# A second PSUM bank for the attention's output in the first half of a kernel

## The chip, the cores and the metric

The kernel runs on one core of a Trainium2 chip. The metric is the time on the device of one execution, in microseconds. In this text PE is TensorE (matmuls), DVE is VectorE, ACT is ScalarE, POOL is GpSimd and SP is the engine that issues the loads and stores.

## What is computed

Three layers follow one another. The first is a decayed linear attention over 4 batches, 8 heads, 768 positions and a head size of 64; the second and third are feed-forward layers over the 3072 tokens that come out of it.

```python
# attention, per batch and head
state = gamma * state + outer(k[t], v[t])
y[t] = q[t] @ state / sqrt(D)
# second layer, x is (3072, 512)
h = x @ w_in                                 # (3072, 1024)
e = exp(h - max(h)); solu = h * e / sum(e)
ln = (solu - mean(solu)) / sqrt(var(solu) + 1e-6) * g_ln
x2 = ln @ w_out                              # (3072, 512)
# third layer
h2 = x2 @ w2_in                              # (3072, 2048)
out = (h2 * cos(h2)) @ w2_out
```

## The kernel before

**Two halves.** The first half computes the attention and the second layer, the second half computes the third layer. The change touches the first half alone. It works on tiles of 128 tokens, six to a batch (TILES), 24 in all, and each tile has all eight heads as four pairs.

**Two parts for each number.** Each operand is split in a high part and a low rest, both of the type that PE multiplies fast. `products` issues three matmuls for each product: high by high, high by low and low by high. Names ending in _h are written by ACT as a copy, names ending in _l by DVE or POOL as the whole less the high part. In the rows L321, L323 and L324 are those three matmuls, whatever the product is, so that the names of the operands tell which product it is.

**The attention of a tile.** SC multiplies queries and keys (operands q and k, 12 matmuls). DVE masks the result into p_m (L1116), ACT copies it to p_h (L786) and DVE subtracts to get p_l (L1123), each for two groups g of two head pairs. DL makes the state's products in `ps_d`. ST (DVE) updates the state s, SH and SL split it. O0 and O1 multiply p by v and, for all but the first tile of a batch, q by the state: that is the output of group 0 and of group 1, 12 matmuls each, 6 for the first tile of a batch. ACT copies each group out of PSUM to x_h (L795) and DVE subtracts from PSUM to get x_l (L1149).

**The second layer of a tile.** L1a and L1b (12 matmuls each, operands w1i and x) make h in two banks. L1a waits for x_l of the tile, and for the step U of the tile before, since the bank of h is read there. DVE takes the maximum (nmax, L1169), ACT the exponential (L813), U on DVE multiplies (L1175). CEN subtracts the mean, T0 and T1 transpose on PE (L627), L2a and L2b (18 and 6 matmuls, operands w1o and z) multiply by w_out, YT transposes the result (L662).

**The order.** Every engine walks the same list of steps, STEP, written out by hand, in which each step has a number of tiles by which it lags. For a middle turn of the loop PE's share of it is SC, T0, L1b, DL, T1, O0, L2a, O1, YT, L2b, after the turn's own L1a. The first turns have lists of their own (`head`), and steps whose tile doesn't exist yet are left out: L2a lags by three turns, so in the turns of tiles 0 and 1 nothing of PE stands between O0 and O1. In these turns ACT and DVE also split the weights of the second layer (step W1: ACT L802 and L808, DVE L1158 and L1163), and DVE does the subtractions that POOL does later (by_dve, q_l at L1107 among them). Each engine takes its instructions strictly in the order of the list, and waits on semaphores.

**The eight banks of PSUM in the first half.** `ps_p` and, in the same two banks, `ps_d`: 0 and 1. `ps_o`: 2. Bank 3: nothing. `ps_h`: 4 and 5. `ps_t`: 6. `ps_y`: 7. In the second half `ps_out` is banks 2 to 7.

**The wait in question.** O0 and O1 write the same bank, so each waits until the x_l of the group before it has been read. The third argument of `wait` from the end is how many counts a tile has, the last the index in the tile; a value that is not positive makes no wait.

```python
g = int(name == "O1")
wait(pe, pl_done, b, t, 2, g)
wait(pe, xl_done, b, t, 2, g - 1)
```

Of the kernel before, what the change touches and what calls it, by code (L numbers as in the profile page):

```python
# [94 lines left out]
def build(nc, qT, kT, kn, vn, consts, w1_in, w1_out, g_ln, w2_in, w2_out, y_scratch, w2_split,  # L95
          w2o_split, out):
    ctx = ExitStack()
    with ctx:
# [2 lines left out]

        bank = ctx.enter_context(nc.psum_tensor("bank", [128, 8, 512], F32))
        ps_p = bank[:, 0:2, :]
        ps_o = bank[:, 2, :]

        ps_d = bank[:, 0:2, :].rearrange("p g (j a n) -> p (g j) a n", j=2, a=2)
        ps_h = bank[:, 4:6, :]
# [103 lines left out]
        xh_done, xl_done = sem("xh_done"), sem("xl_done")  # L211
# [76 lines left out]
        def wait(eng, s, batch, tile, per=1, i=0, per_batch=TILES):  # L288


            value = batch * (per_batch * per) + (tile * per + i + 1)
            if not isinstance(value, int):
                assert value.min_val >= 1
                eng.wait_ge(s, value)
            elif value > 0:
                eng.wait_ge(s, value)
# [20 lines left out]
        def products(eng, dst, terms, first, last_one, read_between=False):  # L317

            n = len(terms)
            for i, (ah, al, bh, bl) in enumerate(terms):  # L320
                eng.matmul(dst, ah, bh, start=first and i == 0, stop=False,  # L321
                           skip_group_check=read_between)
                eng.matmul(dst, ah, bl, start=False, stop=False, skip_group_check=read_between)  # L323
                m = eng.matmul(dst, al, bh, start=False, stop=last_one and i == n - 1,  # L324
                               skip_group_check=read_between)
            return m

        def two_pairs(x):

            return x.rearrange("p (j a t) -> p j a t", j=2, a=2)  # L330
# [216 lines left out]
        def _(pe):  # L547
            def step(name, t, b):
                par = t % 2
                if name == "SC":  # L550
# [6 lines left out]
                    for g in range(2):  # L557
                        wait(pe, pm_done, b, t - 1, 2, g)
                        for j in range(2):
                            p = 2 * g + j  # L560
                            cols = slice(p * C, (p + 1) * C)
                            m = products(pe, ps_p[:, g, j * 256:(j + 1) * 256], [
                                (k_h[:, par, cols], k_l[:, par, cols], q_of(q_h, par, p),
                                 q_of(q_l, par, p))], True, True)
                        m.then_inc(qk_done, 1)
                elif name == "DL" and t % TILES < TILES - 1:
# [3 lines left out]
                    for p in range(PAIRS):  # L570
                        if p % 2 == 0:
# [4 lines left out]
                        m = pe.matmul(ps_d[:, p, 0, :], n_l[:, par, cols], v_h[:, par, cols],  # L576
                                      start=False, stop=True)
                    m.then_inc(d_done, 1)
                elif name in ("O0", "O1"):

                    g = int(name == "O1")
                    wait(pe, pl_done, b, t, 2, g)
                    wait(pe, xl_done, b, t, 2, g - 1)
                    if g == 0:
                        wait(pe, v_lo, b, t)
                        if t % TILES > 0:
# [1 line left out]
                    for j in range(2):  # L588
                        p = 2 * g + j
                        cols = slice(p * 128, (p + 1) * 128)  # L590
                        o = slice(j * 256, (j + 1) * 256)
                        terms = [(v_h[:, par, cols], v_l[:, par, cols],
                                  p_h[:, g, o], p_l[:, g, o])]
                        if t % TILES > 0:
                            n = (t % TILES - 1) % 2
                            terms.append((s_h[:, n, cols], s_l[:, n, cols],
                                          q_of(q_h, par, p), q_of(q_l, par, p)))
                        m = products(pe, ps_o[:, o], terms, True, True)
                    m.then_inc(o_done, 1)
                elif name in ("L1a", "L1b"):  # L600
                    half = int(name == "L1b")
# [3 lines left out]
                    for k in range(KD):  # L605
                        if isinstance(b, int) and t == 0:
                            pe.wait_ge(w1_lo, k + 1)
                        if half == 0 and k % 2 == 0:
                            wait(pe, xl_done, b, t, 2, k // 2)
                        m = products(pe, ps_h[:, half, :], [  # L610
                            (x_h[:, par, k, :], x_l[:, par, k, :],
                             w1i_h[:, k, cols], w1i_l[:, k, cols])], k == 0, k == KD - 1)
# [147 lines left out]
        def _(act):  # L760
# [3 lines left out]
            def step(name, t, b):  # L764
# [8 lines left out]
                elif name == "PQ":  # L773
                    wait(act, q_sc, b, t)
                    for a in range(2):
                        r = slice(64 * a, 64 * a + 64)
                        m = act.copy(q_h[r, par, :, a, :], raw[r, par, 0, :].rearrange(  # L777
                            "p (c t) -> p c t", c=PAIRS))
                    m.then_inc(q_hi, 1)
                elif name == "PN":  # L780
                    wait(act, n_sc, b, t)
                    act.copy(n_h[:, par, :], raw[:, par, 2, :]).then_inc(n_hi, 1)
                elif name == "SC":
                    for g in range(2):
                        wait(act, pm_done, b, t, 2, g)
                        act.copy(p_h[:, g, :], p_m[:, g, :]).then_inc(ph_done, 1)  # L786
                elif name == "SH" and t % TILES < TILES - 1:
                    wait_state(act, st_done, b, t)
                    act.copy(s_h[:, t % TILES % 2, :], s_32[:, :]).then_inc(sh_done, 1)
                elif name in ("O0", "O1"):  # L790
                    g = int(name == "O1")
                    wait(act, o_done, b, t, 2, g)
                    for a in range(2):
                        r = slice(64 * a, 64 * a + 64)
                        m = act.copy(x_h[r, par, 2 * g:2 * g + 2, :],  # L795
                                     two_pairs(ps_o[r, :])[:, :, a, :])
                    m.then_inc(xh_done, 1)
                elif name == "W1":
                    act.wait_ge(ld_w1[t], 16)
                    w = w1_raw[:, t % W1_SLOTS, :]  # L800
                    if t < KD:
                        act.copy(w1i_h[:, t, :], w).then_inc(w1_hi, 1)  # L802
                    else:

                        act.wait_ge(ld_mask, 32)
                        for n in range(2):
                            k = 2 * (t - KD) + n
                            m = act.activation(w1o_h[:, k, :], w[:, n * 512:(n + 1) * 512],  # L808
                                               ACT.Copy, scale=g_col[:, k:k + 1])
                        m.then_inc(w1_hi, 1)  # L810
                elif name == "EX":
                    wait(act, nm_done, b, t)
                    act.activation(e_b, ps_h[:, :, :].rearrange("p a n -> p (a n)"), ACT.Exp,  # L813
                                   bias=nmax[:, par:par + 1],
                                   accum_out=esum[:, par:par + 1]).then_inc(e_done, 1)
                elif name in ("T0", "T1"):
                    g = int(name == "T1")
                    wait(act, t_done, b, t, 2, g)
                    act.copy(z_h[:, 4 * g:4 * g + 4, :].rearrange("p k t -> p (k t)"), ps_t[:, :])\
                        .then_inc(zh_done, 1)  # L820
                elif name in ("L2b", "LD"):
                    wait(act, l2_done, b, t)
                    wait(act, scl_done, b, t, 2, 1)
                    act.activation(y32, ps_y[:, :], ACT.Copy, scale=scl[:, par, 3:4])\
                        .then_inc(y_done, 1)
                elif name == "SQ":
                    wait(act, nmu_done, b, t)
                    act.activation(e_b, u_b, ACT.Square, bias=nmu[:, par:par + 1],
                                   accum_out=ssq[:, par:par + 1]).then_inc(sq1_done, 1)
                elif name == "WH" and unit(b, t) is not None:  # L830
                    u = unit(b, t)
                    unit_wait(act, s4_done, b, u)
                    unit_wait(act, wi_stored, b, u - 1, 16)
                    act.copy(w_out[:, :, 0, :], w_raw[:, A11:, :]).then_inc(wi_hi, 1)
                    unit_wait(act, ld_wo, b, u, 16)
                    unit_wait(act, wo_stored, b, u - 1, 16)
                    act.copy(wo_out[:, 0, :], wo_raw[:, :]).then_inc(wo_hi, 1)
                elif name == "TBL":
                    act.activation(warm[:, :], mhalf[:, :], ACT.Sin)
                elif name == "YH":  # L840
                    y_hi(0, t)
                elif name == "P":
                    slot(0, 0, t, True)
                elif name == "Q":
                    slot(0, 1, t, True)
# [229 lines left out]
        def _(dve):  # L1075
# [9 lines left out]
            def step(name, t, b):  # L1085
# [58 lines left out]
                elif name in ("O0", "O1"):  # L1144
                    g = int(name == "O1")
                    wait(dve, xh_done, b, t, 2, g)
                    for a in range(2):
                        r = slice(64 * a, 64 * a + 64)
                        m = dve.tensor_tensor(x_l[r, par, 2 * g:2 * g + 2, :],  # L1149
                                              two_pairs(ps_o[r, :])[:, :, a, :],  # L1150
                                              x_h[r, par, 2 * g:2 * g + 2, :].bitcast(F32),
                                              ALU.subtract)
                    m.then_inc(xl_done, 1)
# [261 lines left out]
```

## Time and profile before

| what | value |
|---|---|
| time, median of 3 runs | 953.51 us (953.22 to 953.98) |
| the profiled execution's own time | 953.76 us |
| its span in the profile | 952.0 us |
| PE busy | 924.0 us, 97% |
| DVE busy | 714.0 us, 75% |
| ACT busy | 563.1 us, 59% |
| POOL busy | 294.5 us, 31% |
| mean granted clock of PE | 0.991 |

The span runs from the first to the last instruction that the profile records; 1.76 us of the execution's own time lie around it. An engine's idle time matters only where the chain of work that ends last passes through it. The granted clock is given as a share of 2.4 GHz: 1.00 is the upper of its two levels, 0.50 is the lower, 1.2 GHz. The end of a matmul in the profile is modelled, and one may start before the record of the one ahead has ended: the distance between two starts tells the pace.

### The profile page before, as it was taken

The page shows a single profiled execution, that of the slowest core. Times are in us where ns is not written, and L with a number is a line of the kernel's source. Part 1 is how long each engine was busy: PE and PEld are TensorE (multiplying, and loading weights), DVE is VectorE, ACT ScalarE, POOL GpSimd, SP SyncE. Part 2 cuts the span into 40 slices and gives each one's busy share as a digit, 9 for nine tenths or more (in the row PEclk, how much of TensorE's full clock was granted, in tenths as well). Part 3 has the DMA queues.
Part 4 walks back from the last instruction along what each step waited for, and adds up shares of the span by engine and source line. Part 5 has one row for each costly group of instructions (what it writes and reads, how often), then busy time and mean ns, then how long its engine had stood idle before and what let it go on. Part 6 is the DMA issues. An engine that isn't in the chain of part 4 may idle for free.

```text
span 952.0 us, 14590 instructions
## 1 busy us (share of the span) xinstructions
PE 924.0 (97%) x4912; PEld 819.3 (86%) x4912; DVE 714.0 (75%) x1052; ACT 563.1 (59%) x923; POOL 294.5 (31%) x282
## 2 busy tenths in 40 slices
PE   3799999999999999999999999999999999999998
PEld 3588888888888888888989999999999999999997
DVE  8989799988998798977656586566766566766564
ACT  5656656657657567546645475555665455656453
POOL 2475777777776767751000000000000000000000
PEclk8799999999999999999999999999999999999999
DMA  7423364453463453528796444734446444454301
GB/s 279 156 67 117 101 228 164 159 174 138 183 228 118 162 191 138 202 85 267 250 314 215 115 123 125 241 111 124 114 127 218 148 118 122 113 184 121 110 12 66
DMA packets 106520, 148.18 MB, mean 156 GB/s; under 512 B 7408, under 2 KB 77040, under 8 KB 106480
## 3 DMA queue, kind: packets, MB, share of 16 engines
q1 hardware_dynamic: 106480, 147.69, 47.7%
q8 instruction: 20, 0.33, 0.1%
q14 instruction: 20, 0.16, 0.1%
HBM read 112.01 MB, written 35.65 MB: 155 GB/s over the span
## 4 chain that ended last, share of the span: by engine, by line
PE 88%; DVE 8%; ACT 2%; issue 1%; DMA 1%; POOL 0%; SPq 0%; DVEq 0%; ACTq 0%; POOLq 0%
PE bank L321 28%; PE bank L324 28%; PE bank L323 28%; PE bank L627 2%; DVE p_l L1123 1%; PE bank L662 1%; DVE p_m L1116 1%; PE bank L574 1%; DVE wo_out L1223 1%; DVE s_l L1142 1%; DVE z_l L1203 1%; ACT q_h L777 1%; DVE nmax L1169 1%; DVE w1i_l L1158 0%; DVE x_l L1149 0%
## 5 line engine op out<-in xcount | busy, mean ns | idle before, releaser
L321 PE MATMUL bank<-yc_h,ring 128*128 128x384 f32 x448 | 151.5, 338 | 0.0
L323 PE MATMUL bank<-yc_l,ring 128*128 128x384 f32 x448 | 151.3, 338 | 0.0
L324 PE MATMUL bank<-yc_h,ring 128*128 128x384 f32 x448 | 150.9, 337 | 0.0
L1049 POOL TENSOR_TENSOR y_raw<-y_raw,t 128x768 f32<-128x768 f32 x4 | 7.4, 1854 | 361.2 <-DVE yc_l L1234 361.2
L1252 DVE SCALAR_TENSOR_TENSOR gg<-turns,c 128x768 f32<-128x768 int32 x64 | 61.0, 953 | 63.8 <-ACT turns L866 63.8
L872 ACT ACTIVATE gg<-gg 128x768 f32<-128x768 f32 x64 | 54.2, 846 | 80.2 <-DVE gg L1259 80.1
L866 ACT ACTIVATE turns<-c 128x768 int32<-128x768 f32 x64 | 54.2, 847 | 79.1 <-DVE c L1322 76.6
L321 PEld LDWEIGHTS bank<-yc_h,ring 128*128 128x128 f32 x448 | 84.2, 188 | 7.9 <-issue 0.5
L323 PEld LDWEIGHTS bank<-yc_l,ring 128*128 128x128 f32 x448 | 84.2, 188 | 7.2
L324 PEld LDWEIGHTS bank<-yc_h,ring 128*128 128x128 f32 x448 | 84.1, 188 | 0.0
L321 PE MATMUL bank<-w1i_h,x_h 128*128 128x512 f32 x192 | 78.5, 409 | 4.3 <-DVE x_l L1149 1.8
L982 POOL TENSOR_TENSOR q_l<-raw,q_h 64x512 fp32r<-64x512 f32 x44 | 56.7, 1289 | 65.9 <-ACT q_h L777 62.2
L321 PE MATMUL bank<-w1o_h,z_h 128*128 128x512 f32 x192 | 76.8, 400 | 0.0
L324 PE MATMUL bank<-w1i_h,x_l 128*128 128x512 f32 x192 | 76.0, 396 | 0.0
L323 PE MATMUL bank<-w1i_l,x_h 128*128 128x512 f32 x192 | 75.6, 394 | 0.0
L324 PE MATMUL bank<-w1o_h,z_l 128*128 128x512 f32 x192 | 75.4, 393 | 0.0
L323 PE MATMUL bank<-w1o_l,z_h 128*128 128x512 f32 x192 | 75.1, 391 | 0.0
L324 PE MATMUL bank<-w2o,glo_l 128*128 128x512 f32 x192 | 75.0, 391 | 0.0
L323 PE MATMUL bank<-w2o,glo_h 128*128 128x512 f32 x192 | 75.0, 391 | 0.0
L323 PE MATMUL bank<-w2o,ghi_h 128*128 128x512 f32 x192 | 74.9, 390 | 0.0
L324 PE MATMUL bank<-w2o,ghi_l 128*128 128x512 f32 x192 | 74.8, 390 | 0.0
L321 PE MATMUL bank<-w2o,glo_h 128*128 128x512 f32 x192 | 74.6, 389 | 0.0
(129 smaller groups left out, 2471.9 us busy)
## 6 DMA issues: line engine op xcount, KB each, us to landing
ring<-w_split SPq DMA_DIRECT2D x224, 256.0 KB, 2.8
w_split<-w_out SPq DMA_DIRECT2D x16, 896.0 KB, 6.4
w2o_split<-wo_out SPq DMA_DIRECT2D x16, 512.0 KB, 5.5
w2o<-w2o_split SPq DMA_DIRECT2D x8, 1024.0 KB, 7.7
raw<-kT SPq DMA_DIRECT2D x24, 256.0 KB, 2.6
raw<-qT SPq DMA_DIRECT2D x24, 256.0 KB, 2.9
raw<-kn SPq DMA_DIRECT2D x24, 256.0 KB, 3.9
raw<-vn SPq DMA_DIRECT2D x24, 256.0 KB, 4.8
```

The lines of the kernel that those rows point to most:

```text
L321: eng.matmul(dst, ah, bh, start=first and i == 0, stop=False, skip_group_check=read_between)
L323: eng.matmul(dst, ah, bl, start=False, stop=False, skip_group_check=read_between)
L324: m = eng.matmul(dst, al, bh, start=False, stop=last_one and i == n - 1, skip_group_check=read_between)
L574: pe.matmul(ps_d[:, p, :, :], n_h[:, par, cols], v_hl[:, :, par, cols], start=True, stop=False)
L627: m = pe.transpose(ps_t[:, k * 128:(k + 1) * 128], c_b[:, (4 * g + k) * 128:(4 * g + k + 1) * 128], ident[:, :])
L662: m = pe.transpose(ps_t[:, k * 128:(k + 1) * 128], y32[:, k * 128:(k + 1) * 128], ident[:, :])
L777: m = act.copy(q_h[r, par, :, a, :], raw[r, par, 0, :].rearrange("p (c t) -> p c t", c=PAIRS))
L866: act.activation(turns[:, r, :], flat(c_32[:, r, :, :]), ACT.Copy, scale=INV_2PI)\
L872: act.activation(gg[:, r, :], gg[:, r, :], ACT.Sin, scale=0.5)\
L982: return pool.tensor_tensor(dst, whole, part.bitcast(F32), ALU.subtract)
L1116: dve.tensor_tensor(two_pairs(p_m[:, g, :]), two_pairs(ps_p[:, g, :]), mask[:, 4 * g:4 * g + 4, :].rearrange("p (j a) t -> p j a t", j=2), ...
L1252: dve.scalar_tensor_tensor(gg[:, r, :], turns[:, r, :], -TWO_PI_HI, flat(c_32[:, r, :, :]), ALU.mult, ALU.add)\
```

## The change

`ps_o` becomes two banks, 2 and 3. Group 0 (O0) stays in bank 2 and group 1 (O1) goes to bank 3. PE's wait now asks for the read of the same group of the tile before, where it asked for the group before. Counted from the start of the run, O of group g of tile t waited for 2t + g reads and waits for 2t + g - 1. ACT and DVE read the bank of their group. Nothing is moved, no instruction is added that does work, no transfer changes.

```diff
-        ps_o = bank[:, 2, :]
+        ps_o = bank[:, 2:4, :]
...
                     wait(pe, pl_done, b, t, 2, g)
-                    wait(pe, xl_done, b, t, 2, g - 1)
+                    wait(pe, xl_done, b, t - 1, 2, g)
...
-                        m = products(pe, ps_o[:, o], terms, True, True)
+                        m = products(pe, ps_o[:, g, o], terms, True, True)
...
-                                     two_pairs(ps_o[r, :])[:, :, a, :])
+                                     two_pairs(ps_o[r, g, :])[:, :, a, :])
...
-                                              two_pairs(ps_o[r, :])[:, :, a, :],
+                                              two_pairs(ps_o[r, g, :])[:, :, a, :],
```

## Rows read from the trace of the kernel before

**Rows 1.** The page, busy time, share of the span and instructions of each engine.
```profile
...
PE 924.0 (97%) x4912; PEld 819.3 (86%) x4912; DVE 714.0 (75%) x1052; ACT 563.1 (59%) x923; POOL 294.5 (31%) x282
...
```

**Rows 2.** The waits of PE: waited for, us in total, times, longest.
```profile
...
PE bank L321 <- DVE x_l L1149: 8.0, 6, 2.9
PE bank L321 <- DVE p_l L1123: 3.8, 5, 1.9
...
```

**Rows 3.** The timeline of PE, 14 to 49 us: start, us, instruction, [idle before <- releaser].
```profile
...
17.05 0.28 PE L324 MATMUL bank<-p_h,v_hl 128*128 128x256 f32 x1
20.28 0.55 PE L321 MATMUL bank<-p_h,v_hl 128*128 128x256 f32 x1 [2.95 <-DVE x_l L1149]
...
22.38 0.55 PE L321 MATMUL bank<-q_h,k_h 128*128 128x256 f32 x1 [0.48 <-issue]
...
28.46 0.50 PE L321 MATMUL bank<-w1i_h,x_h 128*128 128x512 f32 x1 [1.26 <-DVE w1i_l L1158]
...
34.22 0.28 PE L324 MATMUL bank<-q_h,s_l 128*128 128x256 f32 x1
36.60 0.35 PE L321 MATMUL bank<-p_h,v_hl 128*128 128x256 f32 x1 [2.10 <-DVE x_l L1149]
...
39.70 0.79 PE L321 MATMUL bank<-w1i_h,x_h 128*128 128x512 f32 x1 [1.23 <-DVE work L1175]
...
44.44 0.80 PE L321 MATMUL bank<-w1i_h,x_h 128*128 128x512 f32 x1 [1.81 <-DVE x_l L1149]
...
```

**Rows 4.** The timeline of DVE, 14 to 49 us.
```profile
...
15.62 1.28 DVE L1123 TENSOR_TENSOR p_l<-p_m,p_h 128x512 fp32r<-128x512 f32 x2
...
20.77 1.40 DVE L1107 TENSOR_TENSOR q_l<-raw,q_h 64x512 fp32r<-64x512 f32 x2
...
38.41 1.23 DVE L1175 SCALAR_TENSOR_TENSOR work<-bank,work 128x1024 f32<-128x1024 f32 x1
...
```

**Rows 5.** The chain that ended last, 16 to 50 us: start, us, what.
```profile
...
32.48 1.23 DVE nmax L1169
...
40.50 3.11 DVE w1o_l L1163 x2
...
44.44 0.80 PE bank L321
...
46.51 0.43 PE bank L323
...
47.58 0.21 PE bank L323
...
49.84 0.23 PE bank L323
```

**Rows 6.** Busy time of each engine by stretch, then granted clock of PE, DMA share, GB/s.
```profile
...
17.00:20.00 3.00, 0.33 (x3) 0.12 (x2) 2.95 (x5) 2.56 (x6) 1.27 (x1) 0.56 0.59 169
24.00:28.00 4.00, 3.20 (x15) 2.14 (x14) 3.92 (x5) 1.85 (x3) 2.60 (x2) 0.97 0.73 158
34.34:39.70 5.36, 2.03 (x15) 1.61 (x13) 4.62 (x11) 5.29 (x11) 1.04 (x1) 0.83 0.02 5
44.44:48.09 3.65, 3.65 (x11) 3.07 (x12) 3.65 (x6) 1.54 (x3) 0.00 (x0) 0.50 0.70 265
48.09:101.00 52.91, 52.91 (x314) 46.39 (x314) 45.46 (x82) 32.08 (x59) 34.38 (x32) 1.00 0.25 86
...
```

**Rows 7.** The timeline of PE at the first change of batch, 128 to 141 us.
```profile
...
128.92 0.36 PE L321 MATMUL bank<-p_h,v_hl 128*128 128x256 f32 x1 [0.46 <-DVE x_l L1149]
...
140.87 0.39 PE L321 MATMUL bank<-p_h,v_hl 128*128 128x256 f32 x1 [0.43 <-DVE p_l L1123]
```

**Rows 8.** The timeline of DVE, 118 to 142 us.
```profile
...
118.47 1.41 DVE L1116 TENSOR_TENSOR p_m<-bank,cst 128x512 f32<-128x512 f32 x2 [0.47 <-PE bank L324]
...
131.18 0.86 DVE L1149 TENSOR_TENSOR x_l<-bank,x_h 64x256 fp32r<-64x256 f32 x2 [0.88 <-ACT x_h L795]
...
```

**Rows 9.** The timeline of ACT, 126 to 132 us.
```profile
...
130.40 0.75 ACT L795 CAST x_h<-bank 64x256 fp32r<-64x256 f32 x2
...
```

## The prediction

> **What bounds the kernel now.** I read the page first: PE is busy for 924.0 of 952.0 us [rows 1], so the kernel is nearly all PE, and the one thing that a freed wait can win is PE's idle time, 28 us. I read PE's waits next. Of them the x_l that the change speaks of ends six, 8.0 us together, 2.9 the longest; p_l ends five, 3.8 us [rows 2]. The timeline of PE over the first 49 us and around the changes of batch tells which steps these six are [rows 3, 7]:
>
> - O1 of tile 0, started at 20.28 after 2.95 us idle; O1 of tile 1, at 36.60 after 2.10 us.
> - O1 of the first tile of the second batch, at 128.92 after 0.46 us, and the same place one and two batches later, at 234.09 and 339.24 after 0.34 and 0.35 us (these two repeat the pattern).
> - the sixth, 1.81 us before 44.44, is L1a of tile 1. It reads x_l as its operand, which the change leaves as it is.
>
> So the changed wait holds PE for 2.95 + 2.10 + 0.46 + 0.34 + 0.35 = 6.2 us, all in front of O1, none in front of O0. In the other 19 tiles L2a's 18 matmuls stand between O0 and O1 and the bank has been read by then. Last I read what PE waits for next after each of the five places, and in what order DVE and ACT come to it [rows 4, 5, 8, 9]: that decides whether a freed 2.95 us is won or only handed on.
>
> **The change part by part. Tile 0.** O0's last matmul starts at 17.05 [rows 3]; p_l of group 1, the other thing O1 waits for, is done at 15.62 + 1.28 = 16.90 [rows 4]. O1 therefore starts at about 17.2 and not at 20.28. Behind it in PE's queue stands SC of tile 1, which started at 22.38 [rows 3]. It needs q_l of tile 1, which DVE wrote from 20.77 to 22.17 [rows 4]; nothing PE does with O1 comes into DVE's order before that (p_l, weights, state, x_l of group 0, v_l, q_l, back to back), for none of them reads more of PE's work than O0, whose last matmul started at 17.05. So SC starts at 22.38 again. The 2.95 us idle before O1 become idle time after it. Gain: 0.
>
> **Tile 1.** O0's last matmul starts at 34.22 [rows 3] and both p_l were written by 32.48, where DVE begins nmax [rows 5]. O1 starts at about 34.3 instead of 36.60. Behind it stands L1a of tile 1, started at 39.70, and what it waits for is work (U of tile 0, DVE from 38.41, 1.23 us long, so 39.64) [rows 3, 4]. U follows an exponential on ACT and weights on DVE. O1's result is read on ACT behind two weight splits and the copies of q and k rows, and on DVE behind two weight splits that end at 43.61 [rows 5]: none of them was waiting for O1. The chain that ended last goes from nmax at 32.48 through these to L1a's second half at 44.44 with no PE instruction in it [rows 5]. Gain: 0. PE's idle 2.10 and 1.23 us become one of about 3.9.
>
> **The three changes of batch.** At 128.46 O1 could start, and PE runs 0.46 us ahead from there. Its next stall is 0.43 us before 140.87, for p_l [rows 7]. DVE's way to that p_l was last held by PE at 118.47, and after this by ACT alone, 0.88 us before 131.18, for x_h [rows 8]. That x_h is O1's own copy, so here one could hope; but ACT started it at 130.40 with nothing idle before it [rows 9], straight behind n_h, and O1's 6 matmuls, begun at 128.92, were over by then. p_l is ready at the same moment, PE's stall there grows from 0.43 to 0.89 us, and the 0.46 is gone. The other two batches show the same four rows with 0.34 and 0.35 in place of 0.46, and 0.43 before their p_l. Gain: 0.
>
> **The waits themselves.** O0 asks for an older read than before and cannot wait longer. For the very first tile one wait on PE falls away. Bank 3 has no other user in the first half. Nothing is late that was not late, no transfer is issued at another time: the only step that waits for the end of O1 besides its readers is ACT's k_h of the tile two on (L769), and in ACT's list it stands behind the copy of O1, so that wait never decides.
>
> **The clock.** This is the one cost that the trace does not show directly. In its first 49 us PE is granted 1.00 or 0.50. It fell during 17 to 20 (mean 0.56), while O1 of tile 0 was held; it was up again by about 24.2 (0.97 over 24 to 28), 3.9 us after work was resumed at 20.28. It fell again after the halting stretch from 34.34 on (mean 0.83), and rose at 48.09, 3.65 us after L1a resumed at 44.44 [rows 6]. Matmuls of 512 columns start every 0.43 us at the lower level and every 0.23 at the upper one, those of 256 every 0.21 at the lower [rows 5].
>
> With O1 early, PE comes to SC at 22.38 after some 4 us of idling instead of 0.48, so the lower level will hold longer. Taking the two rises above, it ends about 3.7 to 4 us after 22.38, near 26.3. SC takes 12 x 0.21 = 2.6 us and ends at 24.9; three or four matmuls of L1a at 0.43 and the rest at 0.23 bring its first nine to an end at 27.8. The next waits for a weight until 28.46 in any case [rows 3]. The cover is 0.7 us by this. If the level stayed low until 28.46 the nine would end at 24.9 + 9 x 0.43 = 28.8; and L1b has something to spare too: from 28.46 come 15 matmuls, 3.5 us, to 31.95, and nmax takes them at 32.48 [rows 5]. With 0.2 us for the last one to end, 0.3 are left, which cover that. So I take 0, with the upper bound among the rivals. After 39.70 PE's work is placed as before and the level is already the lower one; I take the rise at 48.09 to stay. Were the stretch from 44.44 to 48.09 run at the upper level, its 3.65 us of work would take half: 1.8 us won. A level that stays low for another such stretch costs as much. From 48.09 to 101 PE is never idle [rows 6], and DVE waits for PE at 118.47 [rows 8], so what is won or lost there does carry through to the end.
>
> **The sum** is 0 + 0 + 0 + 0: the profiled execution would take 953.76 us again. It lies 0.25 above the median of the runs, which is the number that I predict: 953.5.
>
> **The rivals. A: the freed waits are won.** If what comes behind O1 were not tied to DVE, 6.2 us would come off: 947.3. The Trainium skill, Perfetto Trace Analysis, section Optimizing Tensor Performance, Matmuls, speaks for it: independent matmul groups should rotate through PSUM banks so that the reading of one overlaps the matmuls of the next. What the rows show is that the overlap will take place and that PE then waits for something else at all five places. Against it speak rows 4, 5 and 8, so I give it 3 in 100. A part of it, the three small waits alone (1.15 us, 952.4), has 5 in 100: it would need one of DVE's or ACT's steps to come earlier with O1.
>
> **B: the clock is up in 44.44 to 48.09.** 951.7, at the edge of what can be told from no change. For it: PE's work is spread otherwise over 17 to 40. Against it: the last 5 us before 44.44 are the same in both. 6 in 100, a third of it beyond the edge.
>
> **C, on the other side: the lower level holds from 22.38 through L1b of tile 0.** PE's work from there to the end of L1b is 12 x 0.21 + 24 x 0.43 = 12.8 us at the lower level, to 35.2, where an end at 32.2 leaves nmax in time. All of DVE and ACT behind nmax would shift by 3.0 us: 956.5. It costs from the point where the level still is the lower one at about 28.8 on, and passes 1.9 us if it is so at 32.9. Against it: PE would have been busy without a pause since 22.38, and from 44.44 to 48.09 it needed 3.65 us of that. 5 in 100; the same sign and nearly the same size has a rise at 48.09 that comes 3.65 us later (955.3), 3 in 100.
>
> **How the numbers follow.** A measurement of this kernel can tell about 0.2%, 1.9 us, from no change: faster is below 951.6, slower above 955.4. My forecast, no change to within the scatter of the runs (0.8 us between the three), has 78 in 100; A 3, its part 5, B 6, C and its like 8. Faster: A and a third of B, 5 in 100. Slower: most of C, 5. Same: 90. The runs may meet the clock's changes at other moments than the profile did, so the range takes in the small sizes of B and C: 952.4 to 954.8. Outside it lie A, most of B and C and a tail of the forecast, under 2 in 10.
>
> **What would show it.** In the changed kernel's timeline of PE: O1 of tile 0 starts near 17.2 and SC of tile 1 at 22.4; O1 of tile 1 near 34.3 and L1a at 39.7; L1a's second half at 44.4. The waits of PE for x_l go from six to one, of 1.8 us, and PE's idle time in the first 49 us stays, now in front of q_l and U. At the three changes of batch no wait before O1, and p_l waits of 0.89, 0.77 and 0.78. The granted clock low from about 17 to 26 instead of 17 to 24. The prediction is wrong if SC of tile 1 or L1a at 39.7 starts earlier, if L1a's last three matmuls start later than 28.6, or if the clock after 44.4 rises at another time than 48.1.

## The result, and the profile after

| | before | after |
|---|---|---|
| median of 19 runs each | 953.60 us (953.08 to 955.01) | 951.93 us (950.22 to 953.58) |
| ratio, 95% interval | | 0.998 (0.9973 to 0.9986) |
| profiled execution's own time | 953.76 us | 953.58 us |
| its span | 952.0 us | 951.8 us |

The change wins 1.67 us at the median (0.17%), where 0 was forecast; 951.93 lies outside the range of 952.4 to 954.8, though not below the 951.6 that the prediction asked of a faster kernel. The profiled execution of the changed kernel is the slowest of its 19, and its median is 1.65 us below. A second set of 11 runs of the same kernel (`again`, below) has its median at 951.95 and its profiled execution at 952.69.

The page of after, the line that answers to [rows 1], and the waits of PE, which answer to [rows 2] (waited for, us in total, times, longest):

```profile
...
PE 923.4 (97%) x4912; PEld 821.7 (86%) x4912; DVE 715.0 (75%) x1052; ACT 563.0 (59%) x923; POOL 294.4 (31%) x282
...
```

```profile
...
PE bank L321 <- DVE q_l L1107: 13.5, 2, 10.3
PE bank L321 <- DVE work L1175: 3.7, 1, 3.7
PE bank L321 <- DVE p_l L1123: 3.1, 4, 1.8
PE bank L321 <- DVE x_l L1149: 2.4, 1, 2.4
PE bank L321 <- DVE w1i_l L1158: 0.8, 1, 0.8
...
```

The waits for x_l went from six to the one that the change leaves alone, and in their place PE waits for q_l a second time and longer for work (3.7 us; before it was 1.2, from 38.47 to 39.70). The timeline of PE of after, in the first 51 us and at the first change of batch, answers to [rows 3, 7]:

```profile
...
17.79 0.41 PE L321 MATMUL bank<-p_h,v_hl 128*128 128x256 f32 x1
...
22.47 0.36 PE L321 MATMUL bank<-q_h,k_h 128*128 128x256 f32 x1 [3.20 <-DVE q_l L1107]
...
28.54 0.50 PE L321 MATMUL bank<-w1i_h,x_h 128*128 128x512 f32 x1 [0.77 <-DVE w1i_l L1158]
...
35.18 0.28 PE L321 MATMUL bank<-p_h,v_hl 128*128 128x256 f32 x1
...
39.77 0.50 PE L321 MATMUL bank<-w1i_h,x_h 128*128 128x512 f32 x1 [3.72 <-DVE work L1175]
...
44.51 0.80 PE L321 MATMUL bank<-w1i_h,x_h 128*128 128x512 f32 x1 [2.41 <-DVE x_l L1149]
...
49.59 0.41 PE L324 MATMUL bank<-q_h,k_l 128*128 128x256 f32 x1
...
128.25 0.39 PE L324 MATMUL bank<-w1o_h,z_l 128*128 128x512 f32 x1
128.48 0.28 PE L321 MATMUL bank<-p_h,v_hl 128*128 128x256 f32 x1
...
140.92 0.39 PE L321 MATMUL bank<-p_h,v_hl 128*128 128x256 f32 x1 [0.42 <-DVE p_l L1123]
```

In the first two tiles it is as forecast: O1 follows O0 at once, and SC of tile 1 (22.47 against 22.38), L1a (39.77 against 39.70) and its second half (44.51 against 44.44) stay where they were. The granted clock does not follow the forecast. The busy times by stretch of after, as in [rows 6]:

```profile
...
17.00:20.00 3.00, 2.27 (x11) 1.97 (x10) 2.95 (x5) 1.93 (x5) 1.37 (x1) 0.50 0.55 179
20.00:24.00 4.00, 1.53 (x11) 1.56 (x12) 3.91 (x6) 3.92 (x7) 0.00 (x0) 0.93 0.29 111
24.00:28.00 4.00, 3.78 (x12) 2.76 (x11) 3.92 (x5) 2.50 (x4) 1.95 (x2) 0.64 0.46 138
...
39.70:44.44 4.74, 2.33 (x6) 1.33 (x6) 4.13 (x9) 4.68 (x10) 3.10 (x3) 0.58 0.04 4
44.44:48.09 3.65, 3.58 (x10) 3.00 (x11) 3.62 (x7) 1.62 (x3) 0.00 (x0) 0.50 0.79 282
48.09:52.00 3.91, 3.91 (x19) 3.69 (x19) 2.12 (x5) 1.83 (x3) 2.98 (x4) 0.66 0.01 2
...
```

The level was the upper one while SC began (its matmuls start 0.12 apart from 22.79 on), fell again during it, and was up by 26.9, which the weight wait before 28.54 covered. The second rise came at about 50.7 instead of 48.09 (mean 0.66 over 48.09 to 52): the last matmul of SC at 49.59 still stands at the lower pace. It put PE 1.26 us behind at 52 us.

**Where the time went.** I laid the two timelines of PE over each other by the first matmul of each SC, after less before, in us:

| SC of before starts at | after | again | only_rest | only_head | only_tile0 | after_fill2 | before_fill2 |
|---|---|---|---|---|---|---|---|
| 64.63 | +1.27 | +0.59 | +0.23 | +0.21 | -0.82 | -0.52 | -0.16 |
| 100.04 | +1.06 | +0.33 | +0.10 | -0.01 | -0.61 | -0.97 | +0.08 |
| 117.56 | +0.17 | -0.55 | -0.78 | -0.90 | -0.63 | -1.49 | +0.06 |
| 152.72 | -0.16 | -0.89 | -1.13 | -0.98 | -0.62 | -2.78 | +0.11 |
| 416.49 | -0.16 | -1.04 | -1.23 | -1.08 | -0.74 | -2.90 | +0.05 |

So the gain is not won at the five places at which the change takes a visible wait away. In after, in again and in the two runs below that free tiles 2 to 4 (only_rest, only_head), the larger part, 0.88 to 0.89 us, is won in one turn, between 100.04 and 117.56. Another 0.33 to 0.35 seems to come by 152.72, over the change of batch, but this depends on where one reads: SC stands behind O1 in PE's queue and O0 behind DVE's p_l. The same shifts read at O0:

| O0 of before starts at (tile) | after | again | only_rest | only_head | only_loop | pool_late | dve_late |
|---|---|---|---|---|---|---|---|
| 88.20 (4) | +1.26 | +0.54 | +0.30 | +0.20 | -0.15 | +1.28 | +0.57 |
| 105.81 (5) | +0.28 | -0.44 | -0.67 | -0.79 | -0.15 | +0.53 | +0.60 |
| 123.42 (6) | +0.18 | -0.55 | -0.78 | -0.89 | -0.28 | +0.43 | +0.48 |
| 140.87 (7) | +0.05 | -0.67 | -0.91 | -1.00 | -1.36 | +0.29 | -0.59 |
| 404.64 (22) | +0.05 | -0.82 | -1.02 | -1.07 | -1.49 | +0.17 | -0.58 |
| 421.47 (23) | -0.16 | -1.04 | -1.23 | -1.08 | -1.70 | +0.16 | -0.79 |

Read so, there are three pieces in after: 0.98 us from tile 4 to tile 5, 0.23 from tile 5 to tile 7, and 0.21 at the last tile, 1.42 together. The second piece owes nothing to the wait freed at the change of batch, for only_head, which keeps that wait, has 0.21. The third is there only where the late tiles are freed: 0.21 to 0.22, against 0.01 in only_head and pool_late. The kernels only_rest to dve_late are explained further down.

**The turn at 104 us.** The timeline of DVE of before around it, then that of POOL:

```profile
...
104.23 3.22 DVE L1123 TENSOR_TENSOR p_l<-p_m,p_h 128x512 fp32r<-128x512 f32 x2
107.38 1.21 DVE L1169 TENSOR_REDUCE nmax<-bank 128x1 f32<-128x1024 f32 x1
```

```profile
...
104.16 1.05 POOL L998 TENSOR_TENSOR raw<-raw,cst 128x512 f32<-128x512 f32 x1
105.17 1.74 POOL L982 TENSOR_TENSOR v_hl<-raw,v_hl 128x512 fp32r<-128x512 f32 x1
...
```

The same two of after:

```profile
...
105.30 2.19 DVE L1123 TENSOR_TENSOR p_l<-p_m,p_h 128x512 fp32r<-128x512 f32 x2
107.41 1.21 DVE L1169 TENSOR_REDUCE nmax<-bank 128x1 f32<-128x1024 f32 x1
```

```profile
...
105.45 1.50 POOL L998 TENSOR_TENSOR raw<-raw,cst 128x512 f32<-128x512 f32 x1
106.91 1.74 POOL L982 TENSOR_TENSOR v_hl<-raw,v_hl 128x512 fp32r<-128x512 f32 x1
```

The two subtractions of p_l read SBUF alone. Where POOL's product of k rows (L998) starts first, by 0.07 us here, the pair takes 3.22 us; where DVE starts first, by 0.15, it takes 2.19 and POOL's product 1.50 instead of 1.05. The Trainium skill, SBUF — State Buffer, section Who interferes with whom, says that a DVE instruction with two SBUF inputs, tensor_tensor among them, contends with a GpSimd instruction that reads SBUF, that the shared port pair is an exclusive lock, and that the order of issue decides who waits. The rows agree: in before POOL ends its product at 104.16 + 1.05 = 105.21 and the first p_l is used at 105.81; two p_l with no such product of POOL beside them took 1.28 us (15.62). In before, PE stood 0.55 us by the profile at 105.81 for this p_l; in after O0 begins at 106.09 with no wait. The whole stall is larger than the 0.55: O0 starts 1.15 us after the start of T1's transposes in before and 0.36 after it in after, 0.79 us less. After began this turn 1.06 us behind and leaves it 0.17 behind.

**Why the order turned.** The wait that the change removes exists in the later tiles too, but no list of waits shows it. The timeline of PE of before at O1 of tile 4:

```profile
...
93.62 0.39 PE L324 MATMUL bank<-w1o_h,z_l 128*128 128x512 f32 x1
94.00 0.36 PE L321 MATMUL bank<-p_h,v_hl 128*128 128x256 f32 x1
...
```

and of after:

```profile
...
94.90 0.39 PE L324 MATMUL bank<-w1o_h,z_l 128*128 128x512 f32 x1
95.12 0.28 PE L321 MATMUL bank<-p_h,v_hl 128*128 128x256 f32 x1
...
```

A 512-column matmul is drawn 0.39 us long while the next one starts 0.23 after it, so a wait of up to 0.16 hides in the drawn length. Before, O1 starts 0.38 after L2a's last matmul, after, it starts 0.22 after it: 0.15 us. O1's second matmul follows the first after 0.19 in before and 0.12 in after, which makes 0.22 us. Of the 22 O1 that follow L2a, 18 start more than 0.25 us after it in before (three of them are the visible waits), 3.53 us in sum over the pace; in after all 22 start after 0.22 or 0.23. At tile 4 the timeline of ACT shows who felt it, before:

```profile
...
95.69 0.74 ACT L795 CAST x_h<-bank 64x256 fp32r<-64x256 f32 x2 [0.16 <-PE bank L324]
...
```

In after the same copy (96.83) has no wait ahead of it. Against before, POOL's product at 105.45 comes 1.29 us late, about as late as PE was ahead of O1 of tile 4 (1.27), while DVE's p_l at 105.30 comes only 1.07 late: DVE has gained 0.22 us on POOL. Some tenths of a us are enough to change who comes first 10 us later.

### The profile page after: what moved, and what is told of

The parts are those of the page before. It is cut to its first block, busy times and chain, and to the rows that moved or that the text cites. A ratio compares the mean times of both kernels' runs of the same rounds, so it can differ in the third digit from the quotient of the medians.

```text
span 951.8 us, 14589 instructions
## 1 busy us (share of the span) xinstructions
PE 923.4 (97%) x4912; PEld 821.7 (86%) x4912; DVE 715.0 (75%) x1052; ACT 563.0 (59%) x923; POOL 294.4 (31%) x282
## 4 chain that ended last, share of the span: by engine, by line
PE 71%; DVE 19%; ACT 4%; issue 4%; DMA 1%; DVEq 0%; POOL 0%; SPq 0%; POOLq 0%
PE bank L321 23%; PE bank L323 23%; PE bank L324 23%; DVE p_l L1123 3%; DVE s_l L1142 2%; DVE wo_out L1223 2%; DVE p_m L1116 2%; ACT q_h L777 2%; DVE z_l L1203 2%; DVE nmax L1169 2%; ACT x_h L795 1%; DVE s L1134 1%; DVE s L1139 1%; PE bank L627 1%; DVE x_l L1149 1%
```

## The experiments

Each ran in five rounds beside the kernel before; medians in us, with the lowest and highest. "Pairs" are the durations of the p_l x2 near 69, 104 and 121 us in the profiled execution: before 3.06, 3.22, 3.21; after 3.06, 2.19, 2.62. Where an expectation speaks of rival theories, they are these, in the order in which I formed them: the time comes from tile 0 or 1 and the clock; it comes from the freed waits of the later tiles as such; it comes from the order in which DVE and POOL start ("who comes first").

**again.** The changed kernel once more.

> The changed kernel once more, for its clocks run by run and a second profile. Theory 1, the clock: the removed wait of O1 of tile 1 lets PE keep the upper level after 39.7 us in many executions, and those take 950.2 to 950.8 us at a mean clock of 0.996 or more; the others take 951.9 to 953.6 at 0.990 to 0.995. Theory 2, the order of work: a gain of 1.7 us that is there in every execution and comes from the places after the changes of batch; then time and mean clock are not tied.

951.95 (950.17 to 952.69, 11 runs), before 953.47, ratio 0.9977 (0.9968 to 0.9986); pairs 3.02, 2.20, 2.62. The gain is real, and the same pairs are short. The two executions at a mean clock of 0.998 took 950.17 and 950.64, as the first theory said, but the other nine, at 0.990 to 0.995, took 951.42 to 952.69, which is less than any execution of before beside them (952.76 to 954.93): the clock is not the whole of it.

**only_tile0, only_tile1, only_rest.** The new bank everywhere, the new wait only in the tiles named:

```python
if isinstance(b, int) and b == 0 and t == 0:   # t == 1; or: not isinstance(b, int) or t > 1
    wait(pe, xl_done, b, t - 1, 2, g)
else:
    wait(pe, xl_done, b, t, 2, g - 1)
```

> Both banks, but only O1 of tile 0 is freed; all other O0 and O1 keep the old wait. Theory 1: the freed work lies between 17 and 20 us, where what follows waits for q_l until 22.4; 953.6 us, no gain, mean clock 0.99. Theory 2: 953.6 as well.

> Both banks, but only O1 of tile 1 is freed. Theory 1: most or all of the gain of the changed kernel, median 951 to 952.5 us, with some executions near 950.5 at a mean clock of 0.996 or more. Theory 2: 953.6, as before.

> Both banks, and all but tiles 0 and 1 are freed: the three places after a change of batch. Theory 1: 953.6 less the 0.2 us by which the rest of the changed kernel's trace runs ahead after 134 us, so 953.3 to 953.6. Theory 2: the whole gain, near 951.9.

Tile 0: 953.44 (953.0 to 953.9), ratio 1.0 (0.9991 to 1.0009), pairs 3.29, 3.21, 3.21. Tile 1: 954.07 (952.99 to 955.03), 1.0005 (0.9996 to 1.0014), pairs 3.16, 3.23, 3.23. The rest: 952.06 (950.57 to 953.19), 0.998 (0.9971 to 0.9989), pairs 3.15, 2.21, 2.62. The waits of 2.95 and 2.10 us, 5.05 of the 6.2 visible, are worth nothing that these runs can tell, and the first theory, which expected 951 to 952.5 of tile 1 alone, falls; the gain is in tiles whose waits are small or hidden.

**bank_only.** The second bank, with the old waits in all tiles.

> Group 1 has bank 3, and every wait is the old one. If the address of the bank did anything by itself, the time would move; both theories say 953.5, with the p_l pairs of 3.1, 3.2 and 3.2 us near 68, 104 and 121 us.

953.49 (953.18 to 956.07), before 953.70, ratio 0.9999 (0.999 to 1.0008), pairs 3.19, 3.21, 3.24. The address does nothing, the wait does it.

**pool_late.** The kernel before, old bank and old wait, with one small multiplication on POOL (128x64, its result unused) ahead of the k rows' product, in the loop's first turn of each later batch:

```python
if not isinstance(b, int) and t == 0:
    pool.tensor_tensor(pad[:, 0:64], cst[:, 0:64], cst[:, 0:64], ALU.mult)
```

> The kernel before, old wait and one bank, and in the loop's first turn of each batch one more small instruction of POOL ahead of its k row product. Theory 3, who comes first: in the kernel before DVE's first p_l near 104 us asks 0.1 to 0.2 us after POOL has begun that product, waits it out, and the second p_l waits out the next one; with the change it asks first and the pair takes 2.2 us instead of 3.2. Then this kernel, in which POOL comes later by 0.1 us or more, has a pair of 2.2 us there, no stall of PE at 105.8, and about 952.7 us (0.5 to 1 us off 953.5) with the wait of O1 still in place. Rival: the pair is shorter only because O1's result was early; then 953.5 or a little above and the stall at 105.8 stays.

952.56 (952.1 to 953.93), before 953.62, ratio 0.999 (0.9981 to 0.9999). The timeline of POOL of this kernel:

```profile
...
105.44 0.29 POOL L999 TENSOR_TENSOR to_bytes<-cst 128x64 f32<-128x64 f32 x1
105.69 1.49 POOL L1000 TENSOR_TENSOR raw<-raw,cst 128x512 f32<-128x512 f32 x1
...
```

and of DVE:

```profile
...
105.52 2.21 DVE L1125 TENSOR_TENSOR p_l<-p_m,p_h 128x512 fp32r<-128x512 f32 x2
...
```

Work for nothing, 0.29 us of it, makes the kernel 1.06 us faster (the interval allows 0.1 to 1.8). None of the change is in it; only the order is. In its trace the turn at 104 us wins 0.75 us and what follows up to tile 7 another 0.24; the 0.22 us of O1 of tile 4 and the 0.21 of the last tile, which need the freed wait, are missing. At 210.67 and 315.77 the same operation shortens the pair from 2.18 and 2.19 us to 1.43 and 1.44, and PE's starts don't move there: a shorter pair is worth something only where PE waits for it.

**dve_late.** The reverse: the changed kernel, with one 0.27 us operation on DVE ahead of p_l in the same turn.

```python
if not isinstance(b, int) and t == -1:
    dve.tensor_scalar(pad[:, 0:84], cst[:, 0:84], 1.0, None, ALU.mult)
```

> The changed kernel with one more small instruction of DVE (about 0.15 us) ahead of p_l in the loop's first turn of each batch. Theory 3: DVE asks after POOL again, the pair near 105 us takes 3.2 us, PE stalls before O0 of tile 5 and the time rises by 0.8 to 1.2 us from 951.95, to about 953. Rival: 952.0 to 952.2, the 0.15 us alone.

952.95 (952.08 to 954.64), before 953.62, ratio 0.9991 (0.9982 to 1.0): its median is 1.0 us above the changed kernel's, for 0.27 us of work, though the runs scatter by 2.6 us. Pairs 3.06, 3.26, 2.13. Its DVE, then its PE:

```profile
...
104.60 0.27 DVE L1122 TENSOR_SCALAR to_bytes<-cst 128x84 f32<-128x84 f32 x1
104.79 3.26 DVE L1125 TENSOR_TENSOR p_l<-p_m,p_h 128x512 fp32r<-128x512 f32 x2
...
```

```profile
...
106.41 0.39 PE L321 MATMUL bank<-p_h,v_hl 128*128 128x256 f32 x1 [0.78 <-DVE p_l L1125]
...
```

POOL's product began at 104.76, 0.03 us before DVE, the pair is long again and PE's stall is back: from tile 4 to tile 5 nothing is won (+0.57, +0.60). But the next pair turned in exchange. DVE, then POOL:

```profile
...
122.14 2.13 DVE L1125 TENSOR_TENSOR p_l<-p_m,p_h 128x512 fp32r<-128x512 f32 x2
...
```

```profile
...
122.19 1.54 POOL L998 TENSOR_TENSOR raw<-raw,cst 128x512 f32<-128x512 f32 x1
...
```

By tile 7 the kernel has won 1.07 us there, and from tile 4 to the last 1.36, nearly what the changed kernel wins (1.42 in after, 1.58 in again); its profiled execution took 952.95, those of the changed kernel 953.58 and 952.69. The same happens at the later changes of batch: PE falls back by 1.0 us at 211.22 and has it again at 246.05. So the order and the stall at 104 us are as expected, but this trace does not carry the 1.0 us between the medians; where the slower executions lose it is open.

**only_head, only_loop.** As only_rest, with the new wait in the turns ahead of the loop, or in the loop and behind it. The expectations call these tiles 2 to 5 and tile 6 on. That is off by one for O1, which lags by one turn: the loop's first turn has O1 of tile 5, so only_head frees tiles 2 to 4, and only_loop tile 5 on.

```python
if isinstance(b, int) and b == 0 and 2 <= t < TILES:   # or: not isinstance(b, int) or t >= TILES
```

> Both banks, but only O1 and O0 of tiles 2 to 5 of the first batch are freed. Theory 3, who comes first: this is enough to bring PE ahead of POOL at the first p_l near 104 us; the pair of p_l there takes 2.2 us instead of 3.2 and the median is 952.5 to 952.8, about 0.9 off. Rival, the waits at the changes of batch carry the gain: 953.5 and the stall at 105.8 stays.

> Both banks, but only tiles 6 and later are freed, which is where the three waits at the changes of batch lie. Theory 3: the stall at 105.8 and the 3.2 us pair stay; a gain of 0.3 to 0.4 us from the first change of batch alone, 953.1 to 953.3. Rival: the whole gain, 952.

Tiles 2 to 4: 952.49 (952.24 to 953.1), before 953.77, ratio 0.9986 (0.9977 to 0.9995), pairs 3.06, 2.20, 2.62. No visible wait is taken away here (that before O1 of tile 6 stays, 0.51 us over the pace), and 1.28 us are won; in the first table -0.90 at 117.56 and hardly more behind it. Freeing the rest as well (only_rest) lowers the median by 0.43 us, or by 0.13 when each is taken against its own before (gains 1.28 and 1.41); in the traces it is the 0.21 us at the last tile.

Tile 5 on: 952.36 (952.02 to 953.5), 0.9986 (0.9977 to 0.9995), pairs 3.05, 3.20, 2.13. I expected 953.1 to 953.3, the small rest alone, and was wrong: the pair near 121 turned instead, and 1.08 us are won from tile 6 to tile 7. DVE of this kernel, then POOL:

```profile
...
121.38 2.13 DVE L1126 TENSOR_TENSOR p_l<-p_m,p_h 128x512 fp32r<-128x512 f32 x2
...
```

```profile
...
121.43 1.54 POOL L1001 TENSOR_TENSOR raw<-raw,cst 128x512 f32<-128x512 f32 x1
...
```

In before POOL starts at 121.60 and DVE at 121.67, so 0.12 us turned it. Behind the freed O1 of tile 5 the wait of DVE for ACT's x_h is 0.11 us shorter (0.99 for 1.10, at 113.71); I read that as the cause and did not try it by itself. The two parts win 1.28 and 1.41, and together (only_rest) 1.41, or 1.52 to 1.67 with tiles 0 and 1: such gains do not add.

**after_fill, before_fill.** What does the clock do? PE is given matmuls for nothing (512 columns, into the bank of YT) in its idle time ahead of L1a of tile 1 and between its halves, in the changed kernel (8 and 5) and in the one before (5 before O1, then 3 and 5).

```python
def idle_work(n):
    for _ in range(n):
        pe.matmul(ps_y[:, :], w1i_h[:, 0, 0:128], w1i_h[:, 0, 0:512], start=True, stop=True)
```

> The changed kernel, and PE multiplies for nothing where it idled before L1a of tile 1 (8 matmuls from about 36 us, 5 more between the halves; results overwritten). Clock part: if the 950.2 to 950.8 us executions are those in which PE kept the upper level from 39.7 on, then nearly all executions now are at a mean clock of 0.996 or more, and near 950.5 us. Rival: the clocks move and the time stays at 952.

> The kernel before, with work for nothing in the same places (5 matmuls while O1 of tile 1 waits, 3 before L1a, 5 between its halves). If the upper level there were enough by itself, 951.5 to 952. From the executions of the kernel before at a mean clock of 0.998, which took 953.2 to 953.4, I expect 953.2 here: the early start is used up again by waits behind the old one-bank order.

After: 952.04 (950.66 to 952.45), 0.998 (0.9971 to 0.9989), pairs 3.04, 2.19, 2.62; the clock still fell (0.72 over 44.44 to 48.09) and only 3 of 11 executions were near 950.8, so it tells little and is not what I expected. Before: 953.61 (953.18 to 953.88), 0.9999, pairs 3.28, 3.21, 3.22, with the clock at 1.00 there: nothing won.

**after_fill2, before_fill2.** The same with 14 and 12, and with 8, 5 and 12.

> The changed kernel with PE kept busy with work for nothing almost all the time from 36 to 44.4 us (14 matmuls before L1a of tile 1, 12 between its halves), so that it should hold the upper level through 44 to 50 us too, where the first filling lost it again. If the executions of 950.2 to 950.8 us are those with that level held, nearly all come out at 950.2 to 950.9. If it is another chance order of DVE and POOL, the time stays spread between 950.5 and 952.5.

> The kernel before with the same filling (8 while O1 of tile 1 waits, 5 before L1a, 12 between its halves). From the executions of the kernel before at mean clock 0.998 and 1.0, 953.2 to 953.7: the start is 1.5 to 2 us earlier, and is given back between 50 and 90 us. If the clock alone were worth 1.8 us, 951.7.

After: 950.83 (950.58 to 951.44, 7 runs), ratio 0.997 (0.9959 to 0.9981), the best version of this study, pairs 2.23, 2.83, 2.13. Before: 953.44 (953.21 to 953.87), ratio 0.9997 (0.9988 to 1.0006), pairs 3.29, 3.22, 3.22. The clock is up in both; busy times by stretch of after_fill2:

```profile
...
44.44:48.09 3.65, 3.54 (x23) 3.28 (x24) 3.62 (x7) 1.62 (x3) 0.00 (x0) 1.00 0.80 274
...
```

Without the change most or all of the clock's gift is given back: only_tile0, whose profiled execution had the upper level there by itself, and before_fill2 are ahead by 1.61 and 0.96 us at the SC of 47.16, and by 0.82 and 0.16 at the next (first table). With the change, the early start turns the pair near 69 too, and then that near 121 (2.13), where 1.08 us are won from tile 6 to tile 7. The timeline of DVE of after_fill2, and of POOL:

```profile
...
68.22 2.23 DVE L1133 TENSOR_TENSOR p_l<-p_m,p_h 128x512 fp32r<-128x512 f32 x2
...
```

```profile
...
68.39 1.50 POOL L1008 TENSOR_TENSOR raw<-raw,cst 128x512 f32<-128x512 f32 x1
...
```

In before_fill2 both start at 68.57, and the pair takes 3.29.

**after_pool3, after_pool4.** Is it the clock or the pair near 69? Two small POOL operations in the changed kernel, meant to put POOL behind DVE there.

```python
for _n in range(2 * (isinstance(b, int) and b == 0 and t == 3)):   # and t == 4
    pool.tensor_tensor(pad[:, 40 * _n:40 * _n + 40], cst[:, 0:40], cst[:, 0:40], ALU.mult)
```

> The changed kernel, no filling, and two small instructions of POOL (about 0.5 us) ahead of its k row product in the turn of tile 3, where DVE's p_l of tile 2 otherwise begins just after it, near 69 us. Theory 3: the pair there takes 2.2 us instead of 3.1 in nearly all executions, whatever the clock did, and the median goes from 952 to 950.7 to 951.2, the time of the 950.2 to 950.8 executions. Rival, those executions owe it to PE's level alone: 952 stays.

> As after_pool3, with the two small instructions of POOL one turn later, in that of tile 4: the k row product near 69 us, which begins just before DVE's p_l of tile 3, is in that turn, and the last try held POOL back near 52 us. Theory 3: the pair of p_l near 69 takes 2.2 us instead of 3.1, and the median is 950.7 to 951.2 with no filling and at any clock. Rival, the executions of 950.2 to 950.8 owe it to PE's level alone: 952.

With t == 3 they acted at 52 us, a turn too early: 951.99 (951.62 to 952.85), 0.9979 (0.997 to 0.9988), pairs 3.11, 2.19, 2.62. It tells something all the same: its profiled execution had the clock at 1.00 over 44.44 to 48.09 and was 1.36 us ahead at 52, and still has a span of 950.0. With t == 4: 951.58 (951.21 to 952.59), before 953.71, 0.9978 (0.9969 to 0.9987), pairs 2.25, 2.82, 2.13, at the low clock. The order is as I wanted and the sign right, the size 0.4 us where about 1 was expected, with overlapping intervals. Pair or clock alone don't give 950.8; both together (after_fill2) do.

**before_pool36, before_pool46.** The same nudges in the kernel before, with pool_late's (one operation of 40 columns) added.

> The kernel before, one bank and the old wait, with POOL later in the turn of tile 3 (about 0.5 us) and in the first turn of each later batch (0.25 us). Theory 3: pairs of 2.2 us near 69 and 104, as in the fastest executions of the changed kernel; 952.56 was the time with the second alone, the first takes 0.5 to 1 us more off: 951.6 to 952.1. Rival: 952.5, nothing more to gain with the old wait.

> The kernel before, one bank and the old wait, with POOL later in the turn of tile 4 and in the first turn of each later batch. Theory 3: pairs of 2.2 us near 69 and 104 and a median of 951.4 to 951.9, better than the changed kernel's, with the wait of O1 in place. Rival: 952.5.

952.24 (951.73 to 954.07), 0.9987 (0.9978 to 0.9996), pairs 2.50, 2.13, 2.62; and 953.06 (952.13 to 953.88), 0.9991 (0.9982 to 1.0), the pair near 121 long (3.22). I expected 951.6 to 952.1 and 951.4 to 951.9. The second is a clear miss: an order set right early moves the engines so that a later one comes out wrong.

## Why the prediction was wrong

- **Tiles 0 and 1, gain 0: right**, in place and in time. SC, L1a and its second half kept their starts to 0.09 us, and freeing these tiles alone gave 953.44 and 954.07.
- **"In the other 19 tiles L2a's 18 matmuls stand between O0 and O1 and the bank has been read by then": wrong**, and this is the step that failed. I took the list of waits for the whole of the waiting. 15 of the 19 O1 waited up to 0.15 us each, under the drawn length of the matmul before. At tile 4 the wait was worth 0.22 us by itself (the turn wins 0.98 us in after and 0.75 in pool_late, which keeps it), and at the last tiles 0.21 more.
- **The durations of DVE's work were taken as fixed.** The prediction looked at how DVE and ACT follow PE and at no row of POOL. Its "p_l is ready at the same moment" was written of the changes of batch; for the other tiles it has no term at all. But the length of p_l depends on whether POOL has started first. At 104 us this is 1.03 us of DVE's time, and 0.79 us of PE's between T1 and O0. pool_late wins 1.06 us with the order alone: this term was missing from the sum, and by the traces of after and pool_late it is 0.75 + 0.24, some 1.0 of the 1.67 us. dve_late, whose median is 1.0 us higher, brings the stall back, but its trace wins the time again at the next pair and doesn't confirm the size. That the freed waits of tiles 2 to 4 turned the pair is shown by only_head (tiles 0 and 1 and the bank alone don't); the way from tile 4 to 104 us, through ACT's x_h, is read from the timelines and was not tried by itself.
- **The changes of batch, gain 0: right in the sum, wrong in the place.** PE's stall for p_l stayed at 0.42 (140.92) instead of growing to 0.89, because the time is handed back earlier, under drawn lengths again. The timeline of PE of after:

```profile
...
135.08 0.28 PE L324 MATMUL bank<-q_h,k_l 128*128 128x256 f32 x1
135.45 0.63 PE L627 MATMUL bank<-ident,work 128*128 128x128 f32 x4
...
139.49 0.23 PE L576 MATMUL bank<-v_hl,n_l 128*128 128x128 f32 x1
139.84 0.66 PE L627 MATMUL bank<-ident,work 128*128 128x128 f32 x4
...
```

T0 starts 0.37 us after the matmul ahead of it, where it is 0.12 in before (135.57, 135.69), and T1 0.35 after. PE, 0.52 us ahead of before behind O1 of tile 6, is 0.24 ahead at T0 and 0.06 behind at T1. The part of rival A to which I gave 5 in 100 did not happen: only_rest and only_head run from tile 5 to tile 7 with 0.24 and 0.21 us won.
- **The freed waits of the steady tiles win nothing until the last**: the distance between the same O1 of two tiles is 17.85 us before (146.67 to 164.52) and 17.84 after (146.58 to 164.42), since O0 then waits longer for p_l. The wait removed became another one, as the prediction had it for the large ones. Only at the last tile does it not come back; before, then after:

```profile
...
421.47 0.36 PE L321 MATMUL bank<-p_h,v_hl 128*128 128x256 f32 x1
...
```

```profile
...
421.31 0.36 PE L321 MATMUL bank<-p_h,v_hl 128*128 128x256 f32 x1
...
```

- **The clock.** "Near 26.3" for the first rise was near (26.9), by luck: the lower level did not hold from 17 on, as forecast, but had given way before SC and fell again during it. "The rise at 48.09 to stay" was wrong in the profiled execution (about 50.7): the 3.65 us of work that came before the rise in the kernel before were 6.2 here. The level differs by execution in both kernels, though. Of the 143 executions of before beside the experiments, the 33 at a mean clock of 0.998 to 1.0 took 953.2 to 954.1 (median 953.6) and the 20 at 0.991 took 953.4 to 954.5 (median 953.7); of rival B's 1.8 us little is left (before_fill2 goes from 0.96 us ahead at 47.16 to 0.08 behind at 100.04, only_tile0 from 1.61 to 0.61 ahead). With the change, 7 of the 19 executions had 0.996 to 0.998 and took 950.2 to 950.8, 9 had 0.990 to 0.995 and took 951.9 to 952.5; three took 953.4 to 953.6, the profiled one among them. That these 7 are what after_fill2 makes regular, an early start and with it the short pair near 69, is my inference: none of them was profiled.

The traces account for 1.42 us of the 1.67: 0.99 by the order, 0.22 at tile 4 and 0.21 at the end. The remaining 0.25 is of the size of the differences between such executions and of the scatter between sets of runs; I cannot assign it.

## What to carry to other kernels

A list of waits that is made from modelled matmul ends hides short ones: compare the distance between starts with the pace of the same shape wherever a semaphore stands. Before a DVE operation with both inputs in SBUF is costed at its duration, look at what POOL does beside it: here the same two subtractions took 1.28 us alone, 2.62 in most tiles, and 2.2 or 3.2 where the two engines started within 0.2 us of each other. There any edit that shifts one of the two engines can move the time by up to 1 us. Where that is suspected, a small useless operation that nudges one engine tests it; look in the trace at whether another place turned at the same time, as in dve_late, and measure several such nudges together, since their gains do not add.

## What the runs showed of the hardware

- The pair of p_l (2 x 128x512) followed the start of POOL's product of k rows in all 456 pairs of the 19 traces: 2.13 to 2.25 us where DVE started 0.03 to 0.20 us first (60 pairs), 3.02 to 3.29 where it started together with POOL or up to 0.26 behind (32), 2.61 to 2.63 where POOL started 0.56 to 0.60 behind DVE or 1.1 ahead (288, most steady tiles), and 1.28 to 1.44 where no such product started within 1.3 us or POOL came at least 0.78 behind (64). The other 12 lie between.
- POOL's product took 1.03 to 1.06 us when it started with DVE's pair or up to 0.79 ahead of it and 1.49 to 1.55 when it came second (and where it started 1.1 ahead), so of the 1.03 us that DVE saves at 104 us POOL pays 0.45.
- The granted clock of the same kernel in the same stretch (17 to 20) was 0.50 in one execution (after) and 1.00 in another (again), with the same work; the mean clock of before's executions ranged from 0.987 to 1.0.
